# A gated complex recurrence with its channels on partitions, its sums in time by scans, and the Fourier stage put between the next batch's chunks

## The reference

```python
mag = np.sqrt(a_re * a_re + a_im * a_im)
scale = np.minimum(mag, 0.999) / (mag + 1e-06)
a_re_n, a_im_n = (a_re * scale, a_im * scale)
for t in range(S):                      # per batch and head, state S is 48 x 48, complex
    ar, ai = (a_re_n[:, :, t, :, None], a_im_n[:, :, t, :, None])
    new_re = ar * S_re - ai * S_im
    new_im = ar * S_im + ai * S_re
    kv = np.einsum('bhd,bhe->bhde', k[:, :, t], v[:, :, t])
    S_re, S_im = (new_re + kv, new_im)
    y[:, :, t] = np.einsum('bhd,bhde->bhe', q[:, :, t], S_re)
```

## Time and profile before

| | us |
|---|---|
| median of 3 runs | 1171.3 (1170.07 to 1179.53) |
| profiled execution, first to last instruction | 1168.7 |
| of it the recurrence and Fourier stages | 0 to 455.8 |
| of it the two channel products | 455.8 to 1168.7 |

### The profile page before, as it was taken

The page is one execution under the profiler, slowest core; times in us unless marked ns, Lnnn a source line. Parts: engine busy times, 40 slices in busy tenths (PEclk is TensorE's granted clock), DMA queues, the critical chain, the costliest instruction groups (busy, mean ns, idle before and its releaser), DMA issues. The chain is left out here.

```text
span 1168.7 us, 17145 instructions
## 1 busy us (share of the span) xinstructions
PE 1072.0 (92%) x6602; PEld 1000.0 (86%) x6602; DVE 524.9 (45%) x830; ACT 386.3 (33%) x631; POOL 147.3 (13%) x98
## 2 busy tenths in 40 slices
PE   1589999999999985699999999995999999999998
PEld 0279579678958984599999999995999999999998
DVE  5689568656956614643342432125331331421411
ACT  6666547445653323212211121115310310311310
POOL 3252044033213201300000000004000000000000
PEclk9889999997999978699999999998999999999999
DMA  9810920572403122430211102000100100100000
GB/s 178 199 21 1 176 69 0 111 125 48 74 7 122 41 81 85 158 134 21 67 40 39 55 27 81 22 14 9 41 21 22 41 20 13 47 20 13 7 21 21
DMA packets 153293, 66.94 MB, mean 57 GB/s; under 512 B 127521, under 2 KB 151457, under 8 KB 153250
## 3 DMA queue, kind: packets, MB, share of 16 engines
q1 hardware_dynamic: 153250, 66.36, 22.6%
HBM read 52.19 MB, written 14.16 MB: 57 GB/s over the span
## 5 line engine op out<-in xcount | busy, mean ns | idle before, releaser
L1162 ACT ACTIVATE hh<-mbank 128x384 fp32r<-128x384 f32 x192 | 94.5, 492 | 371.1 <-PE mbank L1346 371.1
L1255 DVE SCALAR_TENSOR_TENSOR hl<-mbank,hh 128x384 fp32r<-128x384 f32 x192 | 107.1, 558 | 201.1 <-ACT hh L1162 201.1
L1344 PE MATMUL mbank<-nTh,w1h 128*128 128x384 f32 x576 | 194.0, 337 | 0.7 <-DVE w1l L1277 0.7
L1346 PE MATMUL mbank<-nTh,w1l 128*128 128x384 f32 x576 | 193.4, 336 | 0.0
L1345 PE MATMUL mbank<-nTl,w1h 128*128 128x384 f32 x576 | 193.3, 336 | 0.0
L1344 PE MATMUL mbank<-w2h,hh 128*128 128x384 f32 x576 | 193.1, 335 | 0.0
L1346 PE MATMUL mbank<-w2h,hl 128*128 128x384 f32 x576 | 192.4, 334 | 0.0
L1345 PE MATMUL mbank<-w2l,hh 128*128 128x384 f32 x576 | 192.4, 334 | 0.0
L1344 PEld LDWEIGHTS mbank<-nTh,w1h 128*128 128x128 f32 x576 | 108.9, 189 | 1.5 <-issue 1.5
L1345 PEld LDWEIGHTS mbank<-nTl,w1h 128*128 128x128 f32 x576 | 108.9, 189 | 0.0
L1346 PEld LDWEIGHTS mbank<-nTh,w1l 128*128 128x128 f32 x576 | 108.8, 189 | 0.0
(11 more groups left out here) (146 smaller groups left out, 1662.9 us busy)
## 6 DMA issues: line engine op xcount, KB each, us to landing
w_raw<-in_a_re SPq DMA_DIRECT2D x24, 192.0 KB, 3.6
w_raw<-in_a_im SPq DMA_DIRECT2D x24, 192.0 KB, 3.8
x_early<-in_q SPq DMA_DIRECT2D x24, 192.0 KB, 4.0
w_early<-in_k SPq DMA_DIRECT2D x24, 192.0 KB, 4.4
w_early<-in_v SPq DMA_DIRECT2D x24, 192.0 KB, 4.5
u_scratch<-y_sb SPq DMA_DIRECT2D x24, 192.0 KB, 1.9
w_raw<-in_moe_w_ch SPq DMA_DIRECT2D x2, 2304.0 KB, 8.4
x_early<-u_scratch SPq DMA_DIRECT2D x4, 1152.0 KB, 6.6
```

The costliest lines, as they stand in the source:

```text
L1162: nc.scalar.activation(hh[:, m, :], mm_bank[(g * (KF + TPG) + m) % 2][:, 0:TG], ACT.Relu).then_inc(h_high, 1)
L1255: nc.vector.scalar_tensor_tensor(out=hl[:, m, :], in0=mm_bank[(g * (KF + TPG) + m) % 2][:, 0:TG], scalar=0.0, in1=hh[:, m, :].bitcast(fp32 ...
L1344: nc.tensor.matmul(out, lh, rh, start=(n == 0), stop=False)
L1346: last = nc.tensor.matmul(out, ll, rh, start=False, stop=(n == len(pairs) - 1))
```

## The change

Channels lie on partitions and time runs along the free side. The 384 channels stand as 3 groups of 128, so a stretch of three chunks is 128 x 3 x 384. The work is cut in parts: batch 0 has parts of 1, 2 and 3 chunks, each later batch two of 3; nine in all, with two sets of buffers (`p.s`). The inputs arrive in this layout from the host, in rows of up to 1536 bytes.

- Sums in time are scans on DVE (`tensor_tensor_scan`): nine for logs (one for each group and chunk, L403), nine for phases (L441). The triangular products and their tables are gone.
- q and k are scaled and turned in this layout, a whole part at a time (DVE L452, L458, L459; POOL L591, L597, L598), written to DRAM and read back as 96 rows x 8 heads x time (`turn_over`). No q transposes are left on the PE; k, which the state needs with time on partitions, is transposed from kT (L625) and copied to `kt` by ACT (L302). The chunk's decays go through DRAM as well.
- The gate's steps of a part are spread over the chunks that are 4, 3 and 2 chunks ahead of its first one (k = 0, 1, 2 in `slice_at`).
- A y tile is transposed one chunk after it is made. The Fourier stage of a batch runs between the next batch's chunks: middle row and first width product at chunk j = 1, the others at j = 2, two sequence products at each of j = 3, 4, 5; the additions follow at j = 4, 5 and the next batch's 0. Batch 3's stage remains at the end.
- The batches are written out without a loop.

The diff, cut to its core:

```diff
-            def log_factors(b, i):
-                mm(x_banks[i % 2][:, 0:DM], mx[:, :], lnm[:, i, :], start=True, stop=True).then_inc(x_made, 1)
-            def running_phase(b, i, gates=None):
...
-            def transposes(b, i):
...
+        spans = [(0, 0, 1), (0, 1, 2), (0, 3, 3)] + [(b, j, 3) for b in range(1, B) for j in (0, 3)]
+        parts = [Part(n, *x) for n, x in enumerate(spans)]
+        slice_at = {p.first - 4 + k: (p, k) for p in parts[2:] for k in range(3)}
...
+            def turn_over(p):
...
+                sp.wait_ge(vec_step[p.s], vec0[p.n] + 6)
+                for part in range(2):
+                    sp.dma_start(across("d_turn", part), dstage[:, p.s, :, :]).then_inc(d_out[p.s], 16)
+                sp.wait_ge(pool_step[p.s], pool0[p.n] + GP)
+                for part, src in enumerate((t1_b, k_b)):
+                    sp.dma_start(across("k_turn", part)[:, :, 0:p.T], src[p.s][:, :, 0:p.T]).then_inc(k_out[p.s], 16)
+                sp.wait_ge(vec_step[p.s], vec0[p.n] + GV[p.n])
+                for part, src in enumerate((t2_b, q_b)):
+                    sp.dma_start(across("q_turn", part)[:, :, 0:p.T], src[p.s][:, :, 0:p.T]).then_inc(q_out[p.s], 16)
...
+                sp.dma_start(kT[:, p.s, :, 0:p.T], back("k_turn")[:, :, 0:p.T]).then_inc(k_back[p.s], 16)
+                sp.wait_ge(q_out[p.s], (p.turn + 1) * 32)
+                sp.dma_start(qT[:, p.s, :, 0:p.T], back("q_turn")[:, :, 0:p.T]).then_inc(q_back[p.s], 16)
...
+            for m in range(NM):
+                p, k = slice_at.get(m, (None, None))
+                b, j = divmod(m, NCH)
+                if j < NCH - 1:
+                    keys_turned(m)
+                if k == 0:
+                    act.preload_act_table_set("natural_log_exp_and_others")
+                    magnitudes(p)
+                if k == 1:
+                    factors(p)
+                    act.preload_act_table_set("trig_and_small")
+                    arctangents(p)
+                if k == 2:
+                    sines(p)
+                if m:
+                    evacuate_y(m - 1)
+                if k == 0:
+                    inverses(p)
+                if k == 2 and p.n + 1 < len(parts):
+                    squares(parts[p.n + 1])
...
+                for g, i in product(range(3), range(p.chunks)):
+                    log = t1_b[s][:, g, i * CT:(i + 1) * CT]
+                    last = V.tensor_tensor_scan(log, log, bottom[:, :], 0.0, ALU.add, ALU.max)
...
+            def queries(p):
+                s, T = p.s, slice(0, p.T)
+                dve.wait_ge(act_step[s], act0[p.n] + 13)
+                dve.wait_ge(vec_step[s], vec0[p.n] + GV[p.n] - 1)
+                V.tensor_tensor(t2_b[s][:, :, T], q_b[s][:, :, T], re_b[s][:, :, T], ALU.mult)
+                V.tensor_tensor(q_b[s][:, :, T], q_b[s][:, :, T], im_b[s][:, :, T], ALU.mult).then_inc(vec_step[s], 1)
...
+                if j:
+                    advance_state(m - 1)
+                if b and j == 1:
+                    fold_sequence(b - 1)
+                if b and j >= 4:
+                    add_transform(b - 1, 2 * (j - 4))
+                    add_transform(b - 1, 2 * (j - 4) + 1)
...
+                if k == 0:
+                    squared(p)
+                if k == 1:
+                    ends(p)
+                    signs(p)
+                if k == 2:
+                    phases(p, 2)
+                    scaled_queries(p)
+                masked(m)
+                if k == 0:
+                    logs(p)
+                if k == 1:
+                    phases(p, 0)
+                    phases(p, 1)
+                if k == 2:
+                    queries(p)
...
+            for p in parts[2:]:
+                tangents(p)
+                scaled_keys(p)
+                keys(p)
...
+                if j < NCH - 1:
+                    turn_keys(m)
+                if m:
+                    wait_for_outputs(m - 1)
+                    for h in range(ahead):
+                        output(m - 1, h)
+                pe.wait_ge(k_back[p.s], 16 * (p.turn + 1))
+                pe.wait_ge(q_back[p.s], 16 * (p.turn + 1))
+                for h in range(H):
+                    score(m, h)
+                    if m and h + ahead < H:
+                        output(m - 1, h + ahead)
+                pe.wait_ge(v_in[p.s], 16 * (p.turn + 1))
+                if j < NCH - 1:
+                    update(m)
+                if m:
+                    turn_y(m - 1)
...
+                if b and j >= 3:
+                    sequence_transform(b - 1, 2 * (j - 3))
+                    sequence_transform(b - 1, 2 * (j - 3) + 1)
```

More of the change, by code:

```diff
@@ L1 @@
 from contextlib import ExitStack
+from itertools import product
 import concourse.bass as bass
@@ new lines, in _ @@
+            V.memset(ones[:, :], 1.0)
+            V.memset(dstage[:, :, :, :], 1.0)
+            V.memset(least[:, :], 1.0)
+            V.memset(bottom[:, :], LOG_FLOOR).then_inc(consts_set, 1)
+            p0, p1 = parts[0:2]
+            squared(p0)
+            squared(p1)
+            dve.wait_ge(consts_set, 3)
+            logs(p0)
+            logs(p1)
+            ends(p0)
+            signs(p0)
+            phases(p0, 0)
+            scaled_queries(p0)
+            ends(p1)
+            signs(p1)
@@ new lines, in _ @@
+            queries(p0)
+            for i in range(p1.chunks):
+                phases(p1, i)
+            scaled_queries(p1)
+            squared(parts[2])
+            queries(p1)
+            logs(parts[2])
+            dve.wait_ge(tables_in, 2 * 16)
+            for m in range(NM):
+                p, k = slice_at.get(m, (None, None))
+                b, j = divmod(m, NCH)
+                if j:
+                    advance_state(m - 1)
+                if b and j == 1:
+                    fold_sequence(b - 1)
+                if b and j >= 4:
+                    add_transform(b - 1, 2 * (j - 4))
+                    add_transform(b - 1, 2 * (j - 4) + 1)
+                if b >= 2 and j == 0:
+                    add_transform(b - 2, 4)
+                    add_transform(b - 2, 5)
+                if k == 0:
[14 more added lines that the diff above has]
+                    queries(p)
@@ L589, in _ @@
+            for i in range(NT):
+                add_transform(B - 1, i)
             dve.wait_ge(steep_set, 1)
@@ L616, in tiles @@
-            def tiles(b, ahead):
-                pool.wait_ge(qk_in, (b + 1) * 2 * NT * 16)
-                for i in range(NT):
-                    keys(b, i)
-                    if ahead and i == 1:
-                        pool.wait_ge(a_made, (b + 1) * KD)
-                        im_squares(b + 1, next_gates)
-                if ahead:
-                    tangents(b + 1, next_gates)
-            for step in (im_squares, tangents):
-                for g in first_gates:
-                    step(0, g)
@@ L637, in _ @@
+            p0, p1 = parts[0:2]
+            tangents(p0)
+            tangents(p1)
+            scaled_keys(p0)
+            scaled_keys(p1)
+            keys(p0)
+            keys(p1)
+            for p in parts[2:]:
+                tangents(p)
+                scaled_keys(p)
+                keys(p)
         @block.tensor
```

1096 lines of the change are left out of this document (475 added, 621 removed).

## The result

The changed kernel takes 1232.7 us (median of 4 runs, 1229.1 to 1237.9) against 1170.7 us for the kernel before on the same chip: ratio 1.053, 95% interval 1.048 to 1.058. It is 62 us slower, where 26 us less was forecast. The profiled execution spans 1227.2 us.

A forecast was written before the change was run, and what follows sets the result against it. The chain on DVE, ACT and GpSimd was taken to bound each part, 42 us or 46 with Fourier work. The function ends at 347 + 49.7 + 31.9 = 429 against 455.8, giving 1142 + 2.6 = 1145 us, range 1098 to 1186.

The forecast's parts named there:

- It is hidden while a trip takes under 17 us: Trip of q and k through DRAM: 12.5 us plus 5.4 for scores, 18, before DVE wants them at 22.4.
- t = 0: Zero point of one part's chain: where the queries of the part before are rotated, in DVE's program order.
- the trip decides: Rival: the trip through DRAM takes 20 us instead of 12.5, 3 us a part, giving 1163; chance 0.10.
- the PE's clock falls: Rival: PE waits in every part drop its clock to the low level; 1185 at half the work; chance 0.13.
- Nothing else costs: Claim that the next stage's loads still have over 80 us and smaller gate loads were hidden but at the start.
- waits are spread over three chunks: Argument against the clock rival: the PE's waits, near 5 us in each part, are spread over three chunks.
- a scan 0.33 us: Price of one 128-element scan on DVE, 18 in each part, taken near the upper bound of 0.35.
- the turn-taking: Two-input work of DVE and GpSimd adds up; four GpSimd products in each part, 10.6 us, stand beside DVE.
- the chain: Steps of one part on DVE, ACT and GpSimd: 42 us without Fourier work, 46 with it, above the PE's 34.2.
- I am wrong if a part's period is not 42 to 46 us: Test set for the forecast: each us on a part's period is 6 us in the time.
- the lower bound for a scan, 0.21 us: Lowest price of a 128-element scan, from a two-input pass on the L422 rows' line, 0.08 + 128 x 1.04 ns.
- the start: First two parts, one and two chunks, interleaved: first scores some 25 us earlier, part 2's queries done at 75.

The follow-up runs named there:

- e1: The changed kernel with the stores of finished rows issued at the head of the loop's pass, ahead of turn_over and the loads; 1201.5 us.
- e3: e1 with keys and queries of later parts read back early, as old columns, so no score waits for its own part's trip; 1175.6 us.
- e10: e1 with turned keys and queries read back in two pieces, the first chunk's 128 columns first; 1183.7 us.
- e14: e12 with the stores of finished rows back behind turn_over, as in the changed kernel; 1170.4 us.
- e13: e1 with less PE work in the first nine chunks: no products of q with the state, one state update product instead of eight; 1189.0 us.
- e12: e1 with loads held back, first chunk read back first, key products on VectorE and y_turned ahead of the inverses; 1152.4 us.
- e6: e1 with the first keys copied ahead of the third part's squares and the first scores masked ahead of its logs; 1201.8 us.
- e15: e12 with the two moves at the start from e6; 1151.1 us.
- e2: e1 with identity products into an unused bank filling idle PE time at the start and before later parts' first keys; 1204.0 us.
- e9: e1 with the next loads of gates, k and q held back until the part's turned keys and queries have landed; 1197.7 us.

## Why the prediction was wrong

**The step that failed first** is the sum behind "It is hidden while a trip takes under 17 us": 12.5 + 5.4 = 18, against the 22.4 at which DVE wants the scores. From issue to the keys on the chip the trip took 14.8 us, less than 17, and it was not hidden; the term that was most mis-sized is the 5.4 behind it. Measured for part 4 from the end of the queries:

| | forecast | measured |
|---|---|---|
| keys still being made, SP sends them first | 0 | 2.5 |
| issue to read back on chip | 12.5 | 14.8 (4.7 and 10.1) |
| keys turned (not in the sum), outputs and scores, to the masks | 5.4 | 11.6 (1.1 and 10.6) |
| sum | 18 | 28.9 |
| DVE ready for these masks | 22.4 | 26.0 |

The first row depends on where t = 0 lies. The prediction puts it at the end of all four products; from there (183.5) the sum is 26.4 and DVE is ready at 23.5. The second was a read back priced by the earlier trace rows at 6.6 us, which took 9 to 10. The third, 6.2 us too small, is a price at the full clock for work that ran at 0.51 of it, behind the PE's wait of 4.1 us for the keys. The rivals "the trip decides" (0.10) and "the PE's clock falls" (0.13) were the right mechanisms, but they stood side by side, each with too small a price, while the runs show the first setting off the second here: at the end of the stage 5.9 us of waits bring some 9 us of half pace (e1 against e3). Taking the trip out gives 26 us, and first piece first gives 18 (e10).

**What was not in the prediction at all** is SP's queue. I wrote "Nothing else costs", and had not looked at what stands behind `turn_over`'s waits: stores whose landing frees the ring that ScalarE, and by it the PE, waits for. That is 31 us here (e1) and 18 in the shortened kernel (e14). It is half of the 62 us by which the change lost.

**The clock** was priced at 1185 for half of the work. Besides the stretches behind the trips it came true in the parts before the Fourier work, where e13 makes it 9 to 12 us. My argument against it, that waits are spread over three chunks, was no argument: the slow stretch goes on through chunks in which the PE has no gap (14.9 us from 116.68 to 131.60).

**What held**: the PE's durations at the full clock and DVE's (a scan 0.33 us, nine in 2.94; the earlier trace rows for the rest; the half throughput of the Trainium skill, cited in the prediction, fits that row: 2 x 128 x 1.04 ns is 0.27 of the 0.33 us); the turn-taking, 3.78 for 1.35; and the chain, as far as another kernel can show it. In e12, with the trip shortened and the keys on DVE, the rounds of parts 3 to 8 are 44.8 us on average and the shortest 42.4, against 42 to 46 forecast. "I am wrong if a part's period is not 42 to 46 us" was the right test: the periods were 48.4 to 67.9. One slip cost nothing: the lower bound for a scan, 0.21 us, has 0.08 where the two L422 rows leave 0.16 (0.958 - 768 x 1.04 ns), which gives 0.29.

The sum: 1145 + 31 (stores) + 26 (trip, with the pace behind it) + 12 (pace in the first parts) = 1214 of 1232.7. The last two overlap where a slow chunk lies in a round, so this is at most 69 of the 88 us. Part of the rest is in the start (part 2's queries at 83.6, not 75). An earlier start did not help (e6, e15), so what the rest hangs on stays open.

## What to carry to other kernels

When a step moves behind a round trip, write the round out as one loop, with the order of the queue in it, and price each link at the pace the engine has there; a link that is "hidden" by 4 us of slack is not hidden. List what stands behind every wait in a DMA queue and who waits for that. A wait of the PE has a second price, the pace behind it. A small piece of a transfer sent first gave 18 us here, and two engines' shared work put on one of them 21, though neither takes any work away.

## What the runs showed of the hardware

- The PE ran at half pace without a gap in its records: 30 us busy of 30 in e2 (110 to 140), at a granted clock of 0.50, although 26 us of products at full pace had run at the start, with other work and waits in between. The Trainium skill (TensorE: Matmul & The Clock Gate, Part 1: The HAM clock gate) says that activity releases the throttle. These 30 us don't show it, so the clock can't be counted on even where the PE looks full. What brought it back later is not shown.
- The record of the clock can be wrong. In the changed kernel it says 1.00 from 37.7 to 181 us, while eight key transposes take 1.69 us, the time that they take in e2 where the record says 0.50. The same page (Seeing it yourself) calls these events unreliable; the pace of a known instruction decides.
- After waits of 4.0 and 1.9 us the PE took 15.7 us for a chunk's work (e1, 402.90 to 418.61), which took 7.4 without them (e3) and 8.0 with waits of 0.4 each (e10, 390.22 to 398.20).
- A read back of 1152 KB from DRAM right behind its store landed in 9.0 to 10.1 us (medians), against 6.6 for the plain load of the same size and row length in the earlier trace rows. Loads issued behind it made no difference (e9).
- Two loads of 576 KB issued behind the read backs took 10.5 and 11.5 us (e1), and alone 4.3 and 5.7 (e9).
